# Two load queues and a bank per hash chunk in the opening, and a head's sums copied out of PSUM early

## What is computed

```python
# q, k, v: 2 x 8 heads x 768 x 64; proj: 64 x 6
q_bits = (np.einsum('bhsd,dk->bhsk', q, proj) > 0).astype(np.int64)
k_bits = (np.einsum('bhsd,dk->bhsk', k, proj) > 0).astype(np.int64)
q_bucket = np.sum(q_bits * powers, axis=-1)
k_bucket = np.sum(k_bits * powers, axis=-1)
mask = q_bucket[:, :, :, None] == k_bucket[:, :, None, :]
scores = np.where(mask, scale * np.matmul(q, k.transpose(0, 1, 3, 2)), -1000000000.0)
scores = scores - np.max(scores, axis=-1, keepdims=True)
attn = np.exp(scores)
attn = attn / (np.sum(attn, axis=-1, keepdims=True) + 1e-09)
return np.matmul(attn, v).astype(np.float32)
# then: moe (1536 x 512, 8 experts, Sinkhorn gates), moe2 (top-1 routed experts)
```

## Time and profile before

| | |
|---|---|
| Median of 3 runs | 1391.2 us (1391.02 to 1391.27) |
| Profiled execution | 1387.0 us, span 1385.2 us |
| TensorE busy | 1325.8 us, 96% of the span |
| VectorE busy | 877.3 us, 63% |
| ScalarE busy | 585.7 us, 42% |
| GpSimd busy | 296.9 us, 21% |
| Mean granted clock of TensorE | 0.993 |

### The profile page before, as it was taken

The page is one execution under the profiler, slowest core; times in us unless marked ns, Lnnn a source line. Parts: engine busy times, 40 slices in busy tenths (PEclk is TensorE's granted clock), DMA queues, the critical chain, the costliest instruction groups (busy, mean ns, idle before and its releaser), DMA issues.

```text
span 1385.2 us, 25010 instructions
## 1 busy us (share of the span) xinstructions
PE 1325.8 (96%) x9507; PEld 760.7 (55%) x9507; DVE 877.3 (63%) x1555; ACT 585.7 (42%) x909; POOL 296.9 (21%) x210
## 2 busy tenths in 40 slices
PE   6999999798999999999999999999999999999997
PEld 3666666555446545545644554564465455556665
DVE  5999999877557525633743662474275266567984
ACT  6999999753204403411430430232043033225762
POOL 5765666321300300110030030003003000021211
PEclk9999999999999999999999999999999999999999
DMA  8334331114102001101100210110110013268950
GB/s 229 82 88 102 89 80 40 62 42 158 62 24 92 7 1 61 61 0 61 61 0 2 74 45 0 61 61 0 61 61 0 0 62 129 105 215 289 330 203 20
DMA packets 49567, 107.87 MB, mean 78 GB/s; under 512 B 4600, under 2 KB 6776, under 8 KB 49504
## 3 DMA queue, kind: packets, MB, share of 16 engines
q1 hardware_dynamic: 47264, 103.63, 23.2%
q0 software_dynamic: 2240, 3.35, 0.7%
HBM read 93.63 MB, written 17.34 MB: 80 GB/s over the span
## 4 chain that ended last, share of the span: by engine, by line
PE 81%; DVE 10%; issue 4%; ACT 2%; POOL 2%; DMA 1%; SPq 0%; ACTq 0%; DVEq 0%; POOLq 0%
PE ps L1566 14%; PE ps L1569 14%; PE ps L1570 14%; PE ps L1592 10%; PE ps L1594 10%; PE ps L1595 10%; PE ps L1488 2%; DVE probsT_lo L965 2%; DVE row_max L971 2%; ACT probsT_hi L712 1%; PE ps L1498 1%; PE ps L1476 1%; PE ps L1478 1%; DVE x_lo L1043 1%; PE ps L1456 1%
## 5 line engine op out<-in xcount | busy, mean ns | idle before, releaser
L1592 PE MATMUL ps<-x_hi,w_hi 128*128 128x384 f16 x896 | 294.2, 328 | 10.6 <-DVE x_lo L1043 8.9
L1594 PE MATMUL ps<-x_lo,w_hi 128*128 128x384 f16 x896 | 294.3, 328 | 0.0
L1595 PE MATMUL ps<-x_hi,w_lo 128*128 128x384 f16 x896 | 294.2, 328 | 0.0
L1566 PE MATMUL ps<-w_hi,h 128*128 128x512 f16 x768 | 291.0, 379 | 2.3 <-DVE w_lo L1079 2.3
L1570 PE MATMUL ps<-w_hi,h 128*128 128x512 f16 x768 | 291.0, 379 | 0.0
L1569 PE MATMUL ps<-w_lo,h 128*128 128x512 f16 x768 | 291.0, 379 | 0.0
L1199 DVE SCALAR_TENSOR_TENSOR x<-ps,gate_now,x 128x512 f32<-128x512 f32 x84 | 63.1, 751 | 251.8 <-PE ps L1570 250.6
L800 ACT ACTIVATE x1s<-ps 128x384 f32<-128x384 f32 x64 | 30.4, 475 | 326.2 <-PE ps L1595 326.2
L572 POOL TENSOR_TENSOR wf<-wf 128x1024 f32<-128x1024 f32 x8 | 18.9, 2359 | 636.4 <-PE ps L1595 622.0
L821 ACT ACTIVATE h<-parts 128x1152 f16<-128x1152 f32 x64 | 74.4, 1163 | 137.5 <-DVE parts L1157 137.5
L1592 PEld LDWEIGHTS ps<-x_hi,w_hi 128*128 128x128 f16 x896 | 88.2, 98 | 72.0 <-issue 11.7
(11 more groups left out here) (219 smaller groups left out, 2333.3 us busy)
## 6 DMA issues: line engine op xcount, KB each, us to landing
wf<-w1a SPq DMA_DIRECT2D x32, 512.0 KB, 5.8
w_stage_in<-w2a SPq DMA_DIRECT2D x8, 2048.0 KB, 8.8
w_in<-w1b SPq DMA_DIRECT2D x4, 2048.0 KB, 8.6
w_in<-w2b SPq DMA_DIRECT2D x4, 2048.0 KB
w_in_b<-w1b SPq DMA_DIRECT2D x4, 2048.0 KB, 9.9
w_in_b<-w2b SPq DMA_DIRECT2D x4, 2048.0 KB
rows<-blank SPq DMA_DIRECT2D x1, 6682.0 KB, 21.2
qk_in<-qT SPq DMA_DIRECT2D x32, 192.0 KB, 4.0
```

Of the source, the lines that this page charges most:

```text
L1566: first = pe.matmul(acc, a_hi, b_hi, start=(m == 0), stop=False)
L1592: pe.matmul(group_bank(g, role), w_hi, x_hi, start=(opens and kt == 0), stop=False, skip_group_check=not opens)
L1594: pe.matmul(group_bank(g, role), w_hi, x_lo, start=False, stop=False, skip_group_check=not opens)
L1595: last = pe.matmul(group_bank(g, role), w_lo, x_hi, start=False, stop=(kt == 1), skip_group_check=not opens)
```

## The change

In the opening, SP issues the stack, k and then q of head 0, and behind them head 1's stack, V of head 0 and head 1's q and k. ScalarE's queue issues the rest: the patterns and biases, proj twice, and the constants on both sides of the patterns. The three hash chunks of head 0 go to banks 5, 6 and 7, its k patterns to banks 1, 2 and 3, so that TensorE hashes all three one behind the other. ScalarE writes head 0's one-hot rows of q and, at the end, copies the high part of q; VectorE writes the one-hot rows of k.

At the end of heads 0 to 14, VectorE computes the denominator and copies the sums from PSUM into `o_sum`, ahead of the maximum of that step; TensorE's next values wait for that copy (`o_taken`). The reciprocal stays behind the maximum. GpSimd multiplies `o_sum` with the factors into `x_attn`. The last head is finished by VectorE as before.

```diff
--- before.py
+++ after.py
@@ -219,6 +219,7 @@
         probsT_hi = [sb(f"probsT_hi{r}", [P, S], fp16, attn) for r in range(2)]
         probsT_lo = [sb(f"probsT_lo{r}", [P, S], fp16, attn) for r in range(2)]
         denom = sb("denom", [P, QT], fp32, attn)
+        o_sum = sb("o_sum", [P, QT, D], fp32, attn)
         qk_in = [sb(f"qk_in{r}", [P, 2, S], fp32, attn) for r in range(2)]
         A = [sb(f"A{r}", [P, 2, S], fp16, attn) for r in range(2)]
         Q2 = [sb(f"Q2{r}", [P, S], fp16, attn) for r in range(2)]
@@ -255,12 +256,13 @@
 
...
         v_loaded = [sem(f"v_loaded{r}") for r in range(2)]
         qk_loaded = [sem(f"qk_loaded{r}") for r in range(2)]
+        first_q, first_k, patterns_in = sem("first_q"), sem("first_k"), sem("patterns_in")
         stack_loaded = [sem(f"stack_loaded{r}") for r in range(2)]
 
         (w1_loaded, w2_loaded, w1_summed, w1_scaled, w1_hi_ready, w1_lo_ready, w2_hi_ready, w2_lo_ready, xt_turned,
@@ -321,6 +323,14 @@
                 return None
             return 2 * j + heads + 1, c, (heads + 1) % 2, j + (heads + 1) // 2
 
+        def first_bank(c):
+
+            return ps[:, 5 + c, :]
+
+        def first_k_bank(c):
+
+            return ps[:, 1 + c, :]
+
         def x_bank(t):
 
             return ps[:, t if t < QT else 6 + t % 2, :]
@@ -394,14 +404,13 @@
                 sp.dma_start(V_in[r][:, :, :], v_g).then_inc(v_loaded[r], 16)
 
             load_stack(0, 0)
-            sp.dma_start(const[:, :], consts).then_inc(consts_in, 16)
-            sp.wait_ge(zeroed, 1)
-            sp.dma_start(proj2[0:64, 0:NBITS], proj).then_inc(proj_in, 16)
-            sp.dma_start(proj2[64:P, 32:32 + NBITS], proj).then_inc(proj_in, 16)
-            load_qk(0, 0, 0)
+            for half in (slice(0, 64), slice(64, P)):
+                sp.dma_start(qk_in[0][half, 1, :], kT[0]).then_inc(first_k, 16)
+            for half in (slice(0, 64), slice(64, P)):
+                sp.dma_start(qk_in[0][half, 0, :], qT[0]).then_inc(first_q, 16)
             load_stack(1, 1)
+            load_v(0, 0)
             load_qk(1, 1, 0)
-            load_v(0, 0)
             load_v(1, 1)
             sp.dma_start(gates_in[:, :, :], gates).then_inc(gates_loaded, 16)
             w1_of, w2_of = w1a.rearrange("e (t p) f -> e p t f", p=P), w2a.rearrange("e (t p) n -> e p t n", p=P)
@@ -559,9 +568,17 @@
                 pool.tensor_tensor(V_lo[r][:, :, 0:D], V_in[r][:, :, :], V_hi[r][:, :, 0:D], ALU.subtract
                                    ).then_inc(v_split, 1)
 
+            def normalise(g):
+
+                pool.wait_ge(o_taken, g + 1)
+                pool.wait_ge(denom_ready, 2 * g + 2)
+                pool.tensor_tensor(x_pairs[:, g // 2, :, g % 2, :], o_sum[:, :, :],
+                                   denom[:, :].unsqueeze(2).to_broadcast([P, QT, D]), ALU.mult).then_inc(x_ready, 1)
+
             pool.wait_ge(zeroed, 12)
             pool.wait_ge(blank_ready, 1)
             split_v(0, 0, 0)
+            pool.wait_ge(qk_lo, 2)
             split_qk(1, 1)
             split_v(1, 1, 0)
 
@@ -597,9 +614,12 @@
             for j in range(1, G // 2):
                 split_qk(2 * j, 0)
                 split_v(2 * j, 0, j)
+                normalise(2 * j - 2)
                 split_qk(2 * j + 1, 1)
                 split_v(2 * j + 1, 1, j)
+                normalise(2 * j - 1)
                 split_first_w1(j - 1)
+            normalise(G - 2)
             pool.wait_ge(v_split, 3 * G)
 
 
@@ -691,7 +711,7 @@
         @block.scalar
         def _(act):
             def split_k(g, r, turn):
-                act.wait_ge(qk_loaded[r], 64 * turn + 64)
+                act.wait_ge(qk_loaded[r], 64 * turn + 64 * r)
 
                 reached(act, scores_done, QT * g - QT)
                 act.activation(A[r][:, 1, :], qk_in[r][:, 1, :], ACT.Copy).then_inc(qk_hi, 1)
@@ -721,11 +741,28 @@
                 act.activation(K2[r][64:P, cols], psH[64:P, HC:2 * HC], ACT.Identity, bias=k_bias[64:P, :],
                                scale=K_MASK).then_inc(onehot_ready, 1)
 
-            split_k(0, 0, 0)
+            def first_q_buckets(c):
+                act.wait_ge(pattern_done, c + 1)
+                act.activation(Q2[0][64:P, c * HC:(c + 1) * HC], first_bank(c)[64:P, 0:HC], ACT.Relu,
+                               bias=q_bias[64:P, :], scale=Q_MASK).then_inc(onehot_ready, 1)
+
+            patterns_and_bias = slice(C_PATTERN, C_RANK)
+            act.dma_start(const[:, patterns_and_bias], consts[:, patterns_and_bias]).then_inc(patterns_in, 16)
+            act.wait_ge(zeroed, 1)
+            act.dma_start(proj2[0:64, 0:NBITS], proj).then_inc(proj_in, 16)
+            act.dma_start(proj2[64:P, 32:32 + NBITS], proj).then_inc(proj_in, 16)
+            act.dma_start(const[:, 0:C_PATTERN], consts[:, 0:C_PATTERN]).then_inc(consts_in, 16)
+            act.dma_start(const[:, C_RANK:CONST], consts[:, C_RANK:CONST]).then_inc(consts_in, 16)
+            act.wait_ge(first_k, 32)
+            act.activation(A[0][:, 1, :], qk_in[0][:, 1, :], ACT.Copy).then_inc(qk_hi, 1)
+            act.wait_ge(patterns_in, 16)
+            first_q_buckets(0)
+            first_q_buckets(1)
+            act.wait_ge(first_q, 32)
             split_q(0)
-            act.wait_ge(consts_in, 16)
-            for c in range(NHC):
-                one_hot(0, c, 0)
+            first_q_buckets(2)
+            act.wait_ge(qk_hi, 2)
+            act.activation(Q2[0][0:64, :], A[0][0:64, 0, :], ACT.Copy).then_inc(q2_ready, 1)
             split_k(1, 1, 0)
             split_q(1)
 
@@ -947,16 +984,21 @@
 
         @block.vector
         def _(dve):
-            dve.wait_ge(consts_in, 16)
+            dve.wait_ge(patterns_in, 16)
             dve.tensor_copy(patterns[:, :], const[:, C_PATTERN:C_PATTERN + P]).then_inc(setup_ready, 1)
             dve.wait_ge(zeroed, 2)
 
-            def hash_bits(g, c):
+            def hash_bits(g, c, bank=psH):
                 m = NHC * g + c
                 dve.wait_ge(hash_done, m + 1)
                 reached(dve, pattern_done, m)
-                dve.tensor_scalar(bits[0:64, :], psH[0:64, 0:HC], 0.0, None, ALU.is_gt
+                dve.tensor_scalar(bits[0:64, :], bank[0:64, 0:HC], 0.0, None, ALU.is_gt
                                   ).then_inc(bits_ready, 1)
+
+            def first_k_buckets(c):
+                dve.wait_ge(pattern_done, c + 1)
+                dve.tensor_scalar(K2[0][64:P, c * HC:(c + 1) * HC], first_k_bank(c)[64:P, 0:HC], K_MASK,
+                                  k_bias[64:P, :], ALU.mult, ALU.add).then_inc(onehot_ready, 1)
 
             def take_probsT_lo(i, half, r):
 
@@ -970,50 +1012,54 @@
                 dve.wait_ge(scores_done, i + 1)
                 dve.tensor_reduce(row_max[:, slot:slot + 1], psS[r], AX.X, ALU.max
                                   ).then_inc(max_ready, 1)
-                between(0)
+                between()
 
                 dve.wait_ge(max_ready, i + 1)
                 dve.tensor_scalar(row_scale[:, slot:slot + 1], row_max[:, slot:slot + 1],
                                   -0.5 * Q_MASK * K_MASK, EXP_SCALE, ALU.is_gt, ALU.mult
                                   ).then_inc(scale_ready, 1)
-                between(1)
                 dve.wait_ge(scale_ready, i + 1)
                 dve.tensor_scalar(row_bias[:, slot:slot + 1], row_max[:, slot:slot + 1],
                                   row_scale[:, slot:slot + 1], -1.0, ALU.mult, ALU.mult
                                   ).then_inc(bias_ready, 1)
 
-            def sum_up(g, half):
-
-                if half == 0:
-                    dve.wait_ge(pv_done, QT * g + QT)
-                    dve.tensor_scalar(denom[:, :], psO[:, :, D], EPS, V_SCALE, ALU.add, ALU.mult
-                                      ).then_inc(denom_ready, 1)
-                else:
-                    dve.wait_ge(denom_ready, 2 * g + 1)
-                    dve.reciprocal(denom[:, :], denom[:, :]).then_inc(denom_ready, 1)
-
-            def normalise(j, r):
-                g = 2 * j + r
+            def take_o(g):
+
+                dve.wait_ge(pv_done, QT * g + QT)
+                reached(dve, x_ready, g)
+                dve.tensor_scalar(denom[:, :], psO[:, :, D], EPS, V_SCALE, ALU.add, ALU.mult
+                                  ).then_inc(denom_ready, 1)
+                dve.tensor_copy(o_sum[:, :, :], psO[:, :, 0:D]).then_inc(o_taken, 1)
+
+            def invert_sum(g):
+
+                dve.wait_ge(denom_ready, 2 * g + 1)
+                dve.reciprocal(denom[:, :], denom[:, :]).then_inc(denom_ready, 1)
+
+            def normalise_last():
+                g = G - 1
+                dve.wait_ge(pv_done, QT * G)
+                dve.wait_ge(x_ready, g)
+                dve.tensor_scalar(denom[:, :], psO[:, :, D], EPS, V_SCALE, ALU.add, ALU.mult).then_inc(denom_ready, 1)
+                invert_sum(g)
                 dve.wait_ge(denom_ready, 2 * g + 2)
```

(55 more changed lines are left out.)

4 lines of the change are left out of this document (2 added, 2 removed).

## The result

The changed kernel takes 1378.4 us (median of 6 runs, 1375.4 to 1383.0), the kernel before in the same comparison 1391.1 (6 runs, 1388.8 to 1391.8): a ratio of 0.9914, with 95% interval 0.9893 to 0.9935. The forecast was 1384.5, with a range from 1380.5 to 1388.0. The sign was right; the time lies 2.1 us under the range.

What follows compares the result with a forecast made beforehand. VectorE was taken to pace attention, a load-bound chain the opening. From the profiled 1387.0 us, -4.8 (sums) and -1.9 (opening) gave 1380.3; adding the median's 4.2 us offset gave 1384.5, range 1380.5 to 1388.0.

Steps and rivals of the forecast that it cites:

- What bounds attention: Attention loop: VectorE sets the pace, and once a head TensorE makes it wait 0.3 us for scores.
- The sum of part 1: Head changes, sums copied out early: 14 waits of 0.3 us plus one of 0.6 go, 4.8 us gained.
- both bounds: VectorE's copy of the sums out of PSUM: 0.24 us at the lower end, 0.56 at the upper, 0.47 taken.
- The covers: Head changes: denominator's wait on the last values (0.7 us spare) and GpSimd's 0.89 us product both hidden, costing zero.
- rival C: Head change: wait on last values ahead of the maximum stalls VectorE; 1399.5 us at 1.0 us a head; chance 0.04.
- B: Head change: the wait becomes another of 0.3 us, for transposed halves or last values; 1389.3 us; chance 0.08.
- D: Attention: GpSimd's product slows VectorE beside it, costing 3.0 us; 1387.5 us; chance 0.05.
- The opening: Start to first exponential: 16.4 us instead of 18.26, set by head 1's loads; gain 1.9, bounds 1.0 and 2.7.
- T: Opening: start of the first hash, when proj has landed; 4.9 us taken instead of 5.48.
- one of the signs that the prediction named for being wrong: Others: head-change distance not 0.3 us shorter, or first exponential starting after 17.3 us.
- rival A: Opening: gives only 0 to 1.0 us, head 1's loads landing at 15.5 or constants delaying k and q; chance 0.14.
- the MoE stages behind attention I leave as they are: Expert stages after attention: no change, with 1.5 us either way for how they meet the shift, an estimate.

Runs made afterwards that it cites:

- copy_late: Changed kernel with denominator, copy and reciprocal moved behind the maximum and its bias, same operations: 1384.6 us (1 run).
- before: The kernel without the change: 1391.1 us in the first comparison, medians 1389.0 to 1389.7 in the four later series.
- after: The changed kernel itself: 1378.4 us first, 1379.1 in the second series, 1380.9 in the fourth.
- 64 waits: 64 already-met waits ahead of TensorE's first load wait: changed kernel 1381.1 us (ratio 0.9946), kernel before 1391.6 us (1.0018).
- second and fourth series: Repeats of the unchanged changed kernel, each on its own chip against the kernel before: 1379.1 us (ratio 0.9933) and 1380.9 us (0.9940).
- one part alone: Kernel before with only the new opening: 1384.7 us (ratio 0.9977); with only the sums copied out early: 1382.6 us (0.9956).
- after_late: Changed kernel held back by two GpSimd memsets ahead of its first load: 1386.3 us, ratio 0.9979 to the kernel before.

## Why the prediction was right or wrong

**What bounds attention: right.** With the scores there in time VectorE has one wait of 0.2 us in 237, and `copy_late` brings the 14 waits back by the place of VectorE's operations alone.

**The sum of part 1: right, 1.0 us small.** Forecast were 4.8 us, measured 5.8 in the length of attention; the distance of head changes, 0.38 to 0.40 us shorter, gives as much over 15 heads. The copy held VectorE for 0.46 us against 0.47 taken, so the row of the product was the right neighbour; both bounds can go. The term that was off is the denominator: 0.07 us (97.13 to 97.20), not 0.12, and the reciprocal stays hidden, so VectorE's extra work per head fell from 0.59 to some 0.53 instead of staying at 0.59, which is the 0.9 us. By the Trainium skill ("VectorE: DVE Perf Modes", "Why PSUM operands drop a tier") fp32 out of PSUM was to go no faster than 1x, so the copy was to be 0.47; the trace agrees, with 0.46.

**The covers: right.** At a head change the denominator never waits for the last values, so rival C's stall did not appear, nor did B's. The product on GpSimd takes 0.83 us (0.89 taken) beside VectorE's remainders, which take 1.00 us for two against 1.01 before, so D's contention did not appear either: the rule of the Trainium skill ("GPSIMD Engine Reference", "Key points") speaks of two SBUF inputs, and no wide operation of VectorE has them here. The contention itself is real, and the prediction's comparison of two different operations is borne out: in before the sum that takes 2.44 us at 272.19 beside GpSimd takes 0.96 at 305.67, where GpSimd is idle.

**The opening: right in sum, by two errors that did not matter.** The first exponential is 1.6 us earlier in the profile and 2.0 in most others of this kernel, forecast 1.9. T was wrong: the first hash starts at 5.49, not at 4.9, and a first hash at 5.5 was one of the signs that the prediction named for being wrong. The table load does stand behind the issues, as assumed (3.48), but proj, issued at 1.73, takes 3.7 us to land beside the stacks. I had no row for a small load that shares the engines with large ones, and took the issue for the price. The chain behind it was costed 0.2 us too long, so scores came at 13.05 for 12.7. And neither counts, because head 1's load, at 15.0 for 14.7, sets the exponential. This load was issued 1.2 us earlier than before and took 1.5 longer: 6.7 for 5.2. From 5 to 10 us the DMA engines moved 238 GB/s, against 234 with one queue. That agrees with what the Trainium skill states ("DMA: Bandwidth & Descriptors", "Issuing engines are not separate DMA queues"): all issuers run on the same 16 engines, and a second one saves issue time only. The cost that rival A took for it did not come in after's three profiles: head 1's k landed at 14.7 to 15.0, not at 15.5, with V of head 0 ahead of it (with 64 waits added it landed at 15.6).

**The step that failed: "the MoE stages behind attention I leave as they are, with 1.5 us either way", and carrying the 4.2 us between one profile and the median over to the changed kernel.** In the pair of profiles the stages did stay as they were. In the runs they do not. One kernel's executions spread over 8 us: 83 of before lie from 1385.4 to 1394.0 (mean 1389.6, standard deviation 1.9), 18 of after from 1375.4 to 1383.3 (mean 1379.5, deviation 2.5). The 1391.2 from which I set out was the median of three runs that lay high in this spread, and the profile at 1387.0 lay low in it; the difference of 4.2 was no property of the kernel. Pooled, the distance is 10.0 us (12.0 in the first comparison, 10.3 and 8.4 in the second and fourth series), against 7.4 to 7.8 in the steps. So the forecast of 1384.5 was 6.1 us too high for four reasons: 1.6 us in the level of before, 0.9 in the sum, about 2.4 that come from behind attention, and 1.1 because the six runs of the result lay below after's pooled mean, which is luck.

The spread goes with the granted clock: executions of after at a mean clock of 0.994 or 0.995 took 1375.4 to 1378.1 us, at 0.989 or 0.990 1380.2 to 1383.3. The profiles show three places behind attention. One is the first expert's pause for x_lo. In after, 3.2 us long, and the windows behind it:
```profile
306.40 0.32 PE L1639 MATMUL ps<-x_hi,w_hi 128*128 128x384 f16 x1 [3.22 <-DVE x_lo L1089]
```
```profile
308.00:310.00 2.00, 1.28 (x5) 0.62 (x6) 2.00 (x2) 0.00 (x0) 2.00 (x1) 0.50 1.05 360
310.00:312.00 2.00, 1.77 (x7) 0.60 (x6) 2.00 (x3) 0.49 (x1) 0.07 (x1) 0.50 1.06 376
312.00:314.00 2.00, 2.00 (x8) 0.99 (x7) 0.62 (x1) 0.00 (x0) 0.00 (x0) 0.50 1.06 363
314.00:316.00 2.00, 2.00 (x13) 1.13 (x12) 0.72 (x2) 1.25 (x2) 0.00 (x0) 0.94 1.06 376
```
And the same kernel again, whose pause is as long (3.21) and ends at 305.98:
```profile
306.00:308.00 2.00, 2.00 (x6) 0.68 (x6) 2.00 (x1) 0.19 (x1) 2.00 (x2) 0.50 1.06 353
308.00:310.00 2.00, 1.66 (x7) 0.66 (x6) 2.00 (x2) 0.07 (x1) 1.64 (x1) 0.68 1.04 367
310.00:312.00 2.00, 1.40 (x9) 0.91 (x10) 2.00 (x3) 0.42 (x1) 0.00 (x0) 1.00 1.06 377
```
The lower level holds some 7 us in the one and some 3.5 in the other, and the eight dense experts take 892.2 and 890.6 us. Half speed for some 3.4 us longer costs 1.7, about that difference. The second place is where the routed experts begin, near 1250 us in after: pauses of 1.84 and 1.42 us there were followed by a stretch at 0.50 in after, while 1.95 and 1.42 us were followed by none in the same kernel again. Before has such a stretch at 1261 us, and the profiles of one part alone have none, which is most of their 1.5 and 1.9 us. The third is the "issue" pause near 1290 us, from 1.6 to 5.4 us long in these kernels. The clock fell behind pauses of 1.9 us and held behind others of 2.3, so the length of a pause alone does not decide.

**What stays open.** Between the 7.6 us of the steps and the 10.0 of the pooled runs lie about 2.4 us (standard error some 0.6). A part is clock: its recorded mean was 0.9921 over the 18 runs of after and 0.9914 over the 77 of before in the series, and as 0.001 of it goes with 1.0 to 1.1 us within either kernel, this is some 0.7 us (an estimate from these runs); why the clock differs is not shown. The start time was tried and falls (`after_late` adds its delay in full). The position of the other engines' code was tried and doesn't carry it. TensorE's code length moves the time of before by 2 us, and the change alters that code too, so a part may be luck in its length. Against this, with 64 waits in both kernels they are again 10.0 us apart in their means, where the openings and attention of their profiles give 7.0. Some may still be sampling, since the last series was at 8.4. That series ran on another chip than the second; before's means agree to 0.5 us over the four chips, but whether the surplus depends on the chip was not tried. The runs do not separate these.

**What the range lacked.** The bounds of the unknown costs were covered, but not the place from which they were counted. A forecast from 1389.6 instead of 1391.2, with the sum of 6.7, would have been 1382.9, with the scatter of a median on both sides of it: nearer, but still 3.4 us above after's pooled mean.

## What to carry to other kernels

When one engine sets the pace and waits once per round for another, look at what its own code holds back: here a move of 0.5 us of VectorE's work by one instruction, to ahead of the maximum, gave 5.8 us in 15 heads, and the offload that came with it nothing. In an opening, cost the chain of loads first: here either of two repairs gave most of the gain, since the next late step, a load bound by bandwidth, stood close behind. And before a forecast of half a per cent, ask how far one kernel's executions lie apart and where in that spread the profile and the median stand; three runs do not tell.
